# Reordering the first steps of a software-pipelined attention and MoE kernel, with two blocks' transfers issued by ScalarE

## The reference

```python
scores = scale * np.matmul(q_c, k_full.transpose(0, 1, 3, 2))
a = np.exp(scores - max); a = a / (sum(a) + 1e-09)
out[:, :, c_start:c_end] = np.matmul(a, v_full)      # chunks of 32 queries
...
h = x @ w_in                                          # 3072 x 512 @ 512 x 1024
solu = h * softmax(h)
ln = (solu - mu) / np.sqrt(var + 1e-06) * g_ln
x2 = ln @ w_out                                       # 3072 x 1024 @ 1024 x 512
...
e_idx = np.argmax(x2 @ w_gate, axis=1)
out[mask] = gate_w * eom * (np.maximum(x2[mask] @ w1[e], 0.0) @ w2[e])
```

## Time and profile before

| | |
|---|---|
| time, median of 3 runs | 714.68 us (713.56 to 715.36) |
| profiled execution | 714.06 us, of which the span from the first to the last instruction 712.4 us |
| TensorE matmul busy | 681.9 us, 96% of the span |
| VectorE, ScalarE, GpSimd busy | 478.3, 349.9, 183.5 us (67%, 49%, 26%) |
| mean granted TensorE clock | 0.991 of full |
| chain of work that ended last | 83% TensorE, 5% VectorE, 4% DMA, 3% ScalarE |

### The profile page before, as it was taken

The page is one execution under the profiler, slowest core; times in us unless marked ns, Lnnn a source line. Parts: engine busy times, 40 slices in busy tenths (PEclk is TensorE's granted clock), DMA queues, the critical chain, the costliest instruction groups (busy, mean ns, idle before and its releaser), DMA issues.

```text
span 712.4 us, 16271 instructions
## 1 busy us (share of the span) xinstructions
PE 681.9 (96%) x5062; PEld 586.5 (82%) x5063; DVE 478.3 (67%) x777; ACT 349.9 (49%) x783; POOL 183.5 (26%) x376
## 2 busy tenths in 40 slices
PE   7798989999999999999999989999999999999985
PEld 7577889899899899899988877888888888888873
DVE  5877888888888888887646465436575758483332
ACT  3554666666666666665324453226362636352220
POOL 3211335445311111111301312122222223132221
PEclk9999999999999999999999999999999999999997
DMA  8916886877775775642264859426778787733320
GB/s 326 322 33 139 245 224 190 218 204 196 185 166 149 185 169 148 168 115 76 77 194 139 239 159 252 112 78 184 224 173 237 182 220 206 191 92 75 87 60 23
DMA packets 65700, 118.59 MB, mean 166 GB/s; under 512 B 8702, under 2 KB 41726, under 8 KB 65536
## 3 DMA queue, kind: packets, MB, share of 16 engines
q1 hardware_dynamic: 43872, 84.62, 43.7%
q10 hardware_dynamic: 15840, 16.52, 10.3%
q0 software_dynamic: 5952, 16.98, 7.8%
HBM read 73.78 MB, written 14.09 MB: 123 GB/s over the span
## 4 chain that ended last, share of the span: by engine, by line
PE 83%; DVE 5%; DMA 4%; ACT 3%; issue 2%; ACTq 1%; SPq 1%; POOLq 0%; DVEq 0%
PE banks L1395 74%; PE banks L1431 3%; PE banks L1413 2%; DMA r_quads<-r_sb 2%; PE banks L1544 1%; ACTq L808 1%; DMA q_sb<-q_t 1%; DVE hmax L1028 1%; ACT prob L697 1%; PE banks L1591 1%; DVE uT_lo L1011 1%; DMA u_quads<-u_sb 1%; DMA prob_quads<-prob 0%; ACT uT_hi L745 0%; PE banks L1567 0%
## 5 line engine op out<-in xcount | busy, mean ns | idle before, releaser
L1395 PE MATMUL banks<-slots_hi_lo,rT_hi 128*128 128x512 f32 x464 | 147.5, 399 | 2.8 <-DVE rT_lo L1208 2.0
L1395 PE MATMUL banks<-slots_hi_lo,xsT_hi 128*128 128x512 f32 x464 | 124.5, 390 | 2.7 <-DVE xsT_lo L1198 2.5
L1395 PEld LDWEIGHTS banks<-slots_hi_lo,xsT_hi 128*128 128x128 f32 x464 | 86.7, 188 | 21.7 <-issue 3.9
L1395 PEld LDWEIGHTS banks<-slots_hi_lo,rT_hi 128*128 128x128 f32 x464 | 85.5, 190 | 20.2 <-issue 3.5
L1395 PE MATMUL banks<-slots_hi_lo,rT_lo 128*128 128x512 f32 x232 | 91.2, 393 | 0.0
L1395 PE MATMUL banks<-wout_hi,uT_hi 128*128 128x264 f32 x384 | 81.3, 293 | 2.5 <-DVE probT L1007 1.3
L1395 PE MATMUL banks<-wout_hi,uT_lo 128*128 128x264 f32 x384 | 77.9, 284 | 0.0
L1395 PE MATMUL banks<-wout_lo,uT_hi 128*128 128x264 f32 x384 | 77.9, 284 | 0.0
L1208 DVE TENSOR_TENSOR rT_lo<-banks,rT_hi 128x1024 fp32r<-128x1024 f32 x29 | 35.5, 1225 | 60.0 <-ACT rT_hi L819 58.5
L1198 DVE TENSOR_TENSOR xsT_lo<-banks,xsT_hi 128x512 fp32r<-128x512 f32 x30 | 20.7, 689 | 77.4 <-ACT xsT_hi L779 77.4
L1395 PE MATMUL banks<-slots_hi_lo,xsT_lo 128*128 128x512 f32 x232 | 71.6, 390 | 0.0
(11 more groups left out here) (181 smaller groups left out, 1177.0 us busy)
## 6 DMA issues: line engine op xcount, KB each, us to landing
raw_w<-experts SPq DMA_DIRECT2D x56, 512.0 KB, 5.2
r_quads<-r_sb ACTq DMA_DIRECT2D x104, 128.0 KB, 3.9
u_quads<-u_sb SPq DMA_DIRECT2D x88, 128.0 KB, 3.3
v_sb<-v_win SPq DMA_DIRECT2D x24, 384.0 KB, 5.3
k_sb<-k_win SPq DMA_DIRECT2D x22, 384.0 KB, 4.3
prob_quads<-prob SPq DMA_DIRECT2D x63, 128.0 KB, 3.8
x_rows<-x SPq DMA_DIRECT2D x24, 264.0 KB, 2.1
q_sb<-q_t SPq DMA_DIRECT2D x24, 256.0 KB, 3.4
```

The source lines that it names most:

```text
L1395: ins = mm(o, lhs, rhs(part, k, n), start=(k == first and lhs is not None and part == 0 and parts == (0, 1)), stop=(k == final and parts = ...
```

## The change

In steps 2 to 4 of the written-out start, helper calls are put in another order on VectorE, ScalarE and TensorE. ScalarE gets a helper `quads_p` of its own and issues the transfers of probabilities of blocks 3 and 4; SyncE no longer issues these and, where those of block 3 stood, waits for their landing before it loads q and k of block 5. Step 4 of VectorE is now written out as well, so its loop begins a step later.

On SyncE:

```diff
-            quads_p(At(0, 3))
+            sp.wait_ge(quads_p_s, STRIPES * 16)
             load_qk(At(0, 5))
...
             quads_u(At(0, 2))
-            quads_p(At(0, 4))
             load_qk(At(0, 6))
```

On ScalarE:

```diff
+            def quads_p(b):
+
+                act.wait_ge(prob_s, b.i + 1)
+                if b.i > BY_DMA:
+                    act.wait_ge(pT_s, b.i)
+                for n in range(STRIPES):
+                    act.dma_start(prob_quads[n * 32:(n + 1) * 32, :],
+                                  by_stripe[:, n, :, :].rearrange("p u j -> p (u j)")).then_inc(quads_p_s, 16)
...
             square_u(At(0, 1))
+            quads_p(At(0, 3))
             exp_h(At(0, 2))
-            exp_units(At(0, 4))
             high_u(At(0, 1))
             scale_y(At(0, 0))
             high_x(At(0, 3))
+            exp_units(At(0, 4))
             centre_h(At(0, 2))
+            quads_p(At(0, 4))
             square_u(At(0, 2))
+            exp_units(At(0, 5), range(NU // 2))
             high_u(At(0, 2))
-            exp_units(At(0, 5))
+            exp_units(At(0, 5), range(NU // 2, NU))
```

On VectorE:

```diff
             h_max(At(0, 2))
-            mask_scores(At(0, 4))
-            top_scores(At(0, 4))
             turn_u(At(0, 1))
             turn_p(At(0, 3))
             low_u(At(0, 1))
+            mask_scores(At(0, 4))
+            top_scores(At(0, 4))
+            low_x(At(0, 3))
             weigh_h(At(0, 2))
-            low_x(At(0, 3))
             copy_logits(At(0, 0))
             weigh_probs(At(0, 4))
             mask_scores(At(0, 5))
             top_scores(At(0, 5))
+            h_max(At(0, 3))
             turn_u(At(0, 2))
+            turn_p(At(0, 4))
             low_u(At(0, 2))
-            turn_p(At(0, 4))
-            h_max(At(0, 3))
             weigh_probs(At(0, 5))
             weigh_h(At(0, 3))
             low_x(At(0, 4))
             copy_logits(At(0, 1))
             mask_scores(At(0, 6))
             top_scores(At(0, 6))
-            walk_a(dve, step)
+            turn_p(At(0, 5))
+            turn_u(At(0, 3))
+            h_max(At(0, 4))
+            low_u(At(0, 3))
+            weigh_probs(At(0, 6))
+            weigh_h(At(0, 4))
+            low_x(At(0, 5))
+            copy_logits(At(0, 2))
+            mask_scores(At(0, 7))
+            top_scores(At(0, 7))
+            walk_a(dve, step, begin=5)
```

On TensorE:

```diff
             scores(At(0, 4))
-            product_out(At(0, 0), range(2, 4))
-            pe.wait_ge(shift_s, 5)
-            product_out(At(0, 0), range(4, 6))
-            pe.wait_ge(pT_s, 4)
-            product_out(At(0, 0), range(6, KF))
+            product_out(At(0, 0), range(2, KF))
             attention(At(0, 3))
             product_out(At(0, 1), range(0, HALF))
+            product_in(At(0, 3), range(0, 1))
             scores(At(0, 5))
-            product_in(At(0, 3), range(KD))
+            product_in(At(0, 3), range(1, KD))
```

More of the change, by code:

```diff
@@ L370, in build, with walk_a @@
         block = ctx.enter_context(nc.Block())
-        def walk_a(eng, step):
-            for s in range(4, 6):
+        def walk_a(eng, step, begin=4):
+            for s in range(begin, 6):
                 step(At(0, s))
@@ L482, in quads_p @@
                 sp.wait_ge(prob_s, b.i + 1)
-                if not (isinstance(b.i, int) and b.i == BY_DMA):
-                    sp.sem_inc(score_go_s, 1)
-                    sp.wait_ge(pT_s, b.i)
+                sp.sem_inc(score_go_s, 1)
+                sp.wait_ge(pT_s, b.i)
                 for n in range(STRIPES):
```

## The result

The changed kernel takes 717.20 us (median of 7 runs, 716.28 to 718.39) against 714.68 (713.56 to 716.06): ratio 1.0032, 95% interval 1.0018 to 1.0046. It is slower, by 2.3 us by the ratio and 2.5 by the medians. The prediction said 713.7 with a range of 711.6 to 716.2 and was wrong. The profiled execution took 716.45 us, its span 714.7 (before 714.06 and 712.4), and TensorE is busy 682.7 us (before 681.9).

What follows compares the result with a forecast made beforehand. TensorE, busy 96% of the span, was taken as the bound, its idle holes worth about 5 us. Winning 2.2, losing 2.7, winning 1.7 and losing 0.2 at blocks 3 to 6 saves 1.0: 713.7 us, range 711.6 to 716.2.

Steps and rivals of the forecast that it cites:

- attention(3): TensorE's attention call for block 3, after product_out(0): start at about 60.7 us against 62.90, 2.2 us early.
- attention(4): TensorE's next attention call: the gain is lost behind a new hole of 2.7 us; start 77.6 against 77.06, 0.5 late.
- The clock: TensorE's granted clock in the stretch of the change: to stay at 1.00 throughout.
- rival C: Late landings make a hole of 4.5 us before attention(4), and TensorE's clock falls to 1.2 GHz: 717.9 us; chance 0.12.
- attention(5): TensorE's attention call for block 5: the hole of 1.78 us goes; start 91.3 against 92.53, 1.2 us early.
- attention(6): TensorE's attention call for block 6, after a later division: start 105.0 us, 1.0 early, with a hole of 0 to 0.5.
- The end: Kernel's end: a microsecond won or lost before 94 us should reach it nearly whole, giving 713.7 us.

Runs made afterwards that it cites:

- the late order undone: The changed kernel with block 4's transfers on SyncE, h_max(3) again last, low_u(2) ahead of turn_p(4), high_u(2) ahead of all of block 5's exponentials: ratio 1.0003.

## Why the prediction was wrong

- **attention(3), right.** Forecast 60.7, measured 60.89, released by `low_u(1)`; block 3's landing 4.1.
- **attention(4), the step that failed.** The order of VectorE gave 77.1 and a hole of 2.7; to this I added "a delay of the start by 0.5, nearer to the low end because the issues themselves pace that 8.0". The delay was 1.75 us, the wait of `turn_u(2)`: 2.7 + 1.75 is 4.45, and 4.41 was measured. The landing came at 74.7, at the upper bound that I had worked out as 74.65. The bound, from seven transfers back to back that took 8.0 us, was the best row there was, and I argued it away with the pace of the issues. The seven took 8.0 us here too, though issued in 2.5, so that argument falls: what counts is when the bytes are through, not when they are issued. The Trainium skill, DMA: Bandwidth & Descriptors, "Issuing engines are not separate DMA queues", states that transfers interleave on the same 16 DMA engines whichever engine issued them, and that a second issuer saves only the time of issuing. The runs agree: with two issuers at once the last landing of `u_quads` is 5.4 to 6.2 us in five kernels, 3.7 with one.
- **The clock, wrong as a result.** I forecast 1.00 throughout, and held against rival C that the hole of 1.78 us left it there. Behind 4.41 us it stayed at 0.50 for some 5.6 us and cost 2.5; C had priced it at 1.4, from a stretch of 2.7 us. C named the mechanism and its condition (a landing past 74 us) and had a chance of 0.12. Its 3.2 us late at `attention(6)` is what was measured (109.20 against 105.97), but by luck: its clock was 1.1 too cheap and its other delay, 1.8 against 0.7, as much too dear.
- **attention(5), the hole right, the time wrong.** No hole, but at 95.20 instead of 91.3, all of the delay carried over. The reason given holds in the traces: with the new order of step 4 `low_u(3)` ends 15.7 us behind the start of `attention(4)`, with the loop's order 16.5, and there a hole of 1.44 stood although TensorE was late as well. With the hole before `attention(4)` filled and the clock at 1.00, `attention(5)` followed 13.61 us behind `attention(4)` without a hole (forecast 13.7). The order alone is not enough, though: two other kernels with it had holes of 1.22 and 1.27.
- **attention(6).** A hole of 0.54 (forecast 0 to 0.5) at 109.20 instead of 105.0, nearly all of it carried over.
- **The end.** That a loss before 94 us reaches the end "nearly whole" was off by a third: of 3.5 us at `attention(7)`, 2.35 arrived, the rest going in the passage to the experts. C, with 3.2 at `attention(6)` carried to the end, came to 717.9.

The forecast stood also without the second issuer on thin ground: with all transfers on SyncE the same order still makes a hole of 3.97, since `turn_p(4)` then waits for its own landing and `high_u(2)` stands behind block 5's exponentials. I had put neither in the sum.

## What to carry to other kernels

When transfers are given to a second issuer, write down what each waiting instruction needs landed and what leaves at the same time, and take the upper bound of the landing: the sequence of one issuer was here what kept loads and other transfers out of the way. If a move makes TensorE wait some 2 us or more where it had been busy before, price a slow clock behind it as well (1.5 to 3 us here), as a chance for about 2 us; behind every hole of 3 us and more it came here. And bring the producer of the critical transfer forward before changing who issues it.

## What was unexpected of the hardware

- Of the three transfers of 128 KB the last landed 3.3 us after its issue when they went alone, from either issuer, 4.2 to 4.3 behind four of the same issuer, 5.7 to 5.8 beside four of another, and 7.3 behind loads of another.
- Ahead of `attention(4)` the granted clock fell to 0.50 behind idle stretches of 2.19, 3.27, 3.97, 4.03, 4.41, 4.45, 4.49 and 4.54 us. Behind 3.27 and 3.97 it fell only half a microsecond into the work, so that `attention(4)` took 1.58 and 1.61 us. It stayed at 1.00 behind 1.70 and 2.24, where TensorE had worked on 40 more products just before.
- The length of the hole does not decide it at about 2 us. The same hole of 1.91 or 1.92 us near 690 us, ahead of the same products, was followed by a clock of 0.50 in five traces of the changed orders and by 1.00 in seven others. The hole of 2.18 to 2.22 near 30 us was followed by the slow clock in the kernel before and the changed one, and not in two of the others. One such pair, from the changed kernel and from the one with the late order undone, TensorE and then the windows of 3.5 us behind:

```profile
693.01 0.73 PE L1414 MATMUL banks<-slots_hi_lo,rT_hi 128*128 128x512 f32 x2 [1.92 <-DVE rT_lo L1217]
...
690.44 1.17 PE L1413 MATMUL banks<-slots_hi_lo,rT_hi 128*128 128x512 f32 x2 [1.92 <-DVE rT_lo L1216]
```

```profile
693.00:696.50 3.50, 3.49 (x15) 2.97 (x16) 0.43 (x4) 0.00 (x0) 1.21 (x2) 1.00 0.19 75
...
690.40:693.90 3.50, 3.46 (x8) 2.78 (x9) 0.45 (x4) 0.00 (x0) 1.21 (x2) 0.52 0.18 75
```

In no trace did a hole of 2.90 us or more leave the clock at 1.00. What sorts the shorter ones stays open, and one trace does not show what a kernel does every time.
- Where it fell, the way from `attention(4)` to `scores(6)` took 5.7 to 7.2 us instead of 4.2: the same fall costs 1.5 to 3 us.
